# Attention scores with 128 query tokens per matmul where 64 stood, and a logits fold that takes 128 tokens at once

## The chip, the cores and the metric

The kernel runs on one core of a Trainium2 chip. The metric is device time in microseconds (us) of one launch, a median over runs. Every time below is a time of this one core. TensorE (PE) multiplies matrices, VectorE (DVE) and ScalarE (ACT) work on rows, GpSimd (POOL) does what is given to it beside them, SyncE (SP) issues the transfers. TensorE runs at one of two clock levels, 1.2 or 2.4 GHz; the profile gives the granted clock as a share of the higher one.

## The reference

Three layers, one after another, all in float32. The change lies in the first (the scores) and in how the logits of the second are made out of it.

```
# q, k, v: 8 batches, 8 heads, 576 tokens, 64 wide; pool = 8, so 72 keys
k_p = k.reshape(B, H, 72, 8, 64).mean(axis=3);  v_p likewise
scores = matmul(q, k_p.T) / 8;  attn = softmax(scores)
x = matmul(attn, v_p), heads side by side: 4608 tokens x 512
logits = x @ phi                       # 512 x 32 slots
d = softmax(logits, over tokens);  slot_input = d.T @ x
slot_out[e] = relu(slot_input[e] @ w1[e]) @ w2[e]      # 8 experts, 4 slots each
y = softmax(logits, over slots) @ slot_out
h = y @ w_in;  out = (s * relu(h)**2 + b) @ w_out      # 512 -> 2048 -> 512
```

## The kernel before

The attention part works on 36 units. A unit is 128 queries (partitions) times 8 columns of 72 keys. Batches go in pairs of nine units: the first four and the last four are plain units, which hold four heads of two sets of 128 tokens of one batch; the fifth is "mixed" (`is_mixed(U)`), holds 64 tokens of each of the two batches and all 8 heads. So 32 units are plain and 4 are mixed.

A hand-written schedule has STEPS steps. In step n TensorE does, in this order of the program: the fold of the logits of unit n-5 (`fold_logits`, if that unit closes a pair, `closes_logits`), the scores of unit n-1 (L1706 to L1727), the transposes of the queries of unit n (L1751), the logits of unit n-4 (`logits_of`, L1631 or L1626), the transposes of the normalised weights of unit n-3 (L1772), and then pieces of other work: transposes of pooled keys and values (L1543), value times phi (L1566), sums over tokens (L1663, L1668), their turning (L1682) and weighted values (L1691, L1696). Each engine has its own instruction stream; they meet only at semaphores.

What surrounds the scores: ScalarE copies the transposed queries out of PSUM to `qT` (L877), and `qT_kept` lets the scores begin. TensorE needs `sx_ready` of the unit before, since both use the same two PSUM banks `S_B`. When the scores are there (`s_ready`) VectorE takes the maximum (L1191) and subtracts it (L1237), ScalarE takes the exponential (L948), VectorE the sums (L1230) and reciprocals (L1241), GpSimd multiplies (L823), and TensorE transposes (L1772) two steps later.

The score of one head has a contraction of 64 (the head's width), so two heads lie in the upper and lower 64 rows of the array. Before the change each product also takes only 64 of the unit's 128 tokens: `parts()` gives the two halves, `toks` is `0:64` or `64:128`, the result lies in the upper or lower half of a PSUM bank. A plain unit has 4 x 2 x 2 = 16 products, each with 64 rows by 64 columns of stationary data (queries) and 72 moving columns (keys). In the trace every float32 product is two matmul records and two weight-load records, so a unit shows x32. The profile writes such a tile as `64*64`; `128*128` is the full array.

The fold: the logits of unit pairs come out of `logits_of` as four partial sums on four groups of 32 partitions (`l4`, 128 x 256, or 128 x 128 for a mixed unit). `fold` is an identity repeated four times; `l4.T @ fold` adds the four. Before the change it is done for 64 tokens at a time (`128*64`, 32 moving columns): 4 products for a pair, 2 for a mixed unit. VectorE copies the result (L1182).

After the attention (from 193 us of the span) come the experts (L1840, L1864), the hidden layer and its products (L1898 on, the long loop of L1999, L2000, L2010); this part is not touched.

Of the kernel before, what the change touches and what calls it, by code (L numbers as in the profile page):

```python
# [13 lines left out]
P = 128  # L14
# [4 lines left out]
def pooled_attention_soft_moe_squared_relu_kernel(  # L19
# [23 lines left out]
    B, H, S, HD = q.shape  # L43
    D, SLOTS = phi.shape
    EXPERTS, _, F1 = w1.shape
# [3 lines left out]
    KEYS = S // POOL  # L49
    ROW = POOL * HD  # L50
    PER = SLOTS // EXPERTS
    HALF = P // 2
# [18 lines left out]
    HB = H // 2  # L71
# [42 lines left out]
    with ctx:  # L114
        def sb(name, shape, dt=F32, where=ctx):
            return where.enter_context(nc.sbuf_tensor(name, shape, dt))
# [6 lines left out]
        fold = sb("fold", [P, QUADS, SLOTS])  # L123
# [18 lines left out]
        k_sb = {n: sb(f"k_sb{n}", [P, PH, KEYS], where=att)}  # L142
# [6 lines left out]
        qT = sb("qT", [P, HP, P], where=att)  # L149
# [12 lines left out]
        l4 = sb("l4", [P, L4 + P], where=att)  # L162
# [41 lines left out]
        rows = logits[:, :, :].rearrange("p t s -> p (t s)")  # L204
# [30 lines left out]
        Q_B, S_B, A_B, L_B, B_B, MISC = 0, (1, 2), (3, 4), 5, 6, 7  # L235
        bank = []
# [146 lines left out]
        def is_mixed(U):  # L383
            return U % TPP == MIXED

        def unit_half(U):
            u = U % TPP
            return u % 2 if u < MIXED else (u - MIXED - 1) % 2
# [10 lines left out]
        def l4_cols(U):  # L399
            return slice(L4, L4 + P) if is_mixed(U) else slice(0, L4)  # L400

        def logits_closed(U):

            return sum(closes_logits(o) for o in range(U))
# [144 lines left out]
        def parts():  # L549

            return [(bb, slice(HALF * bb, HALF * (bb + 1))) for bb in range(2)]
# [975 lines left out]
        def _(pe):  # L1527
# [71 lines left out]
            def fold_logits(U):  # L1599

                e = logits_closed(U)
                pe.wait_ge(fold_ready, 2)
                pe.wait_ge(l4_kept, e + 1)
                misc_free("logits", e + 1)
                for j in range(1 if is_mixed(U) else 2):
                    for half, toks in parts():
                        first = P * j + HALF * half
                        last = pe.matmul(bank[MISC][toks, SLOTS * j:SLOTS * (j + 1)], l4[:, l4_cols(U)][:, first:first + HALF],
                                         fold[:, 0, :], start=True, stop=True)
                last.then_inc(lg_ready, 1)  # L1610

            def logits_of(U):
# [87 lines left out]
            for n in range(LAST_LOGITS):  # L1700
                U = n - 5
                if 0 <= U < UNITS and closes_logits(U):
                    keep_warm(n, 1)
                    fold_logits(U)

                U = n - 1  # L1706
                if 0 <= U < UNITS:
                    i, bb = U // TPP, unit_batch(U) % 2
                    pe.wait_ge(qT_kept, U + 1)
                    if U % TPP == 0:  # L1710
                        pe.wait_ge(kT_kept, PIECES * (i + 1))
                    if U:
                        pe.wait_ge(sx_ready, U)
                    if is_mixed(U):
                        for h in range(H):
                            rows = slice(HD * (h % 2), HD * (h % 2 + 1))
                            for bb, toks in parts():
                                last = pe.matmul(bank[S_B[h % 2]][toks, KEYS * (h // 2):KEYS * (h // 2 + 1)], qT[rows, h // 2, toks],
                                                 k_sb[i % 2][rows, H * bb + h, :], start=True, stop=True)
                    else:  # L1720
                        for a in range(HB):
                            for j in range(2):
                                rows = slice(HD * j, HD * (j + 1))
                                for _, toks in parts():
                                    last = pe.matmul(bank[S_B[j]][toks, KEYS * a:KEYS * (a + 1)], qT[rows, a, toks],  # L1725
                                                     k_sb[i % 2][rows, H * bb + HB * unit_half(U) + a, :], start=True, stop=True)
                    last.then_inc(s_ready, 1)  # L1727

                for g in groups_at(n, TOP_AT):
                    keep_warm(n, 2)  # L1730
                    turn_tops(g)
                for g in groups_at(n, ROW_AT):
                    keep_warm(n, 1)
                    spread_tops(g)

                U = n
                if U < UNITS:

                    i, w, j = U // TPP, unit_queries(U), unit_tile(U) % TPP
                    if U % TPP in (0, MIXED, MIXED + 1):  # L1740
                        pe.wait_ge(q_in[w], (16, 16, 32)[w] * (i + 1))
                    if n:
                        pe.wait_ge(qT_kept, n)
                        query_bank_free(n - 1)
                    for a in range(HP):
                        if is_mixed(U):
                            src = qbuf[w][:, 2 * a:2 * a + 2, 0, :].rearrange("p h d -> p (h d)")
                        else:
                            j0 = j % (MIXED + 1)
                            src = qbuf[w][:, HB * unit_half(U) + a, j0:j0 + 2, :].rearrange("p j d -> p (j d)")  # L1750
                        last = pe.transpose(bank[Q_B][:, P * a:P * (a + 1)], src, ident[:, :])  # L1751
                    last.then_inc(qT_ready, 1)
                if n == 0:
                    turn_keys(0, 1, 0)
                    turn_keys(0, 2, 0)

                if n == weights_step(0):
                    values_phi(0, n)
                U = n - 4
                if 0 <= U < UNITS:  # L1760
                    keep_warm(n, 1)
                    logits_of(U)

                U = n - 3
                if 0 <= U < UNITS:
                    keep_warm(n, 2)
                    pe.wait_ge(a_ready, U + 1)
                    for g in range(2):
                        if U:
                            pe.wait_ge(aT_kept, 2 * (U - 1) + g + 1)  # L1770
                        for a in range(HB):
                            last = pe.transpose(bank[A_B[g]][0:KEYS, P * a:P * (a + 1)], ex[:, ex_slot(U), HB * g + a, 0:KEYS], ident[:, :])  # L1772
                        last.then_inc(aT_ready, 1)


                if n:
                    for i, u in pieces_with(key_step, n):
                        turn_keys(i, u, n)
                for i, u in pieces_with(value_step, n):
                    turn_values(i, u, n)  # L1780
                for i in range(PAIRS):
                    if i and n == weights_step(i):
                        values_phi(i, n)
                    for half in range(2):
                        if n == natural_step(i, half):
                            values_natural(i, half, n)
                for g, half in b_halves(n):
                    keep_warm(n, half == 0)
                    token_weights(g, half)
                for g in groups_with(bT_step, n):  # L1790
                    keep_warm(n, 1)
                    turn_weights(g)
                for g in groups_with(sums_step, n):
                    keep_warm(n, 1)
                    weighted_values(g)
# [37 lines left out]
            for e in range(EXPERTS):  # L1833
# [4 lines left out]
                for half in range(2):  # L1838
                    for c in range(DC):
                        last = pe.matmul(bank[2 + half][QUAD * c:QUAD * (c + 1), :], sT[:, c, e, :],  # L1840
                                         wv[:, c, BANK * half:BANK * (half + 1)], start=(e == 0), stop=(e == EXPERTS - 1),
                                         skip_group_check=True)
                last.then_inc(matrix_used, 1)
            turn_c(TURN_AT_H)
            for c in range(F1C):
                if c % (F1C // 2) == 0:
                    pe.wait_ge(h_kept, c // (F1C // 2) + 1)
                    pe.wait_ge(h_kept_dve, c // (F1C // 2) + 1)
                last = pe.matmul(bank[6][:, SLOTS * c:SLOTS * (c + 1)], h_sb[:, P * c:P * (c + 1)], fold[:, 0, :],
                                 start=(c == 0), stop=True, skip_group_check=True)  # L1850
            last.then_inc(hT_psum, 1)

            for e in range(EXPERTS):
# [8 lines left out]
                for c in range(F1C):  # L1862
                    quad = c % QUADS
                    last = pe.matmul(bank[4][QUAD * quad:QUAD * (quad + 1), :], hT[:, c, e, :], wv[:, c, :],  # L1864
                                     start=(e == 0 and c < QUADS), stop=(e == EXPERTS - 1 and c >= F1C - QUADS),
                                     skip_group_check=True)
                last.then_inc(matrix_used, 1)
            turn_c(LAST_TURN)
            for c in range(DC):
                if c % (DC // 2) == 0:  # L1870
                    pe.wait_ge(so_kept, c // (DC // 2) + 1)
                last = pe.matmul(bank[5][:, SLOTS * c:SLOTS * (c + 1)], so_sb[:, P * c:P * (c + 1)], fold[:, 0, :],
                                 start=(c == 0), stop=True, skip_group_check=True)
# [190 lines left out]
```

## Time and profile before

| | |
|---|---|
| time, median of 3 runs | 648.23 us (647.69 to 648.74) |
| the profiled execution | 652.14 us, its span 650.3 us |
| mean granted clock | 0.986 |
| PE busy | 629.7 us (97% of the span) |
| DVE, ACT, POOL busy | 481.5, 448.9, 124.2 us |
| scores of plain units (L1725), busy PE | 25.2 us, x1024 |
| folds (L1608), busy PE | 8.0 us, x144 |

The profile counts an engine as busy while at least one of its instructions is in flight. Matmuls of different array tiles run side by side, and the ends of matmuls are modelled, so a sum of durations says little about TensorE; what counts is how far apart the starts lie. The record of a group in a timeline gives the start of its first instruction, the time to the end of its last, and how many records it has. The last 1.8 us of the profiled time lie outside the span.

### The profile page before, as it was taken

The page shows a single profiled execution, that of the slowest core. Times are in us where ns is not written, and L with a number is a line of the kernel's source. Part 1 is how long each engine was busy: PE and PEld are TensorE (multiplying, and loading weights), DVE is VectorE, ACT ScalarE, POOL GpSimd, SP SyncE. Part 2 cuts the span into 40 slices and gives each one's busy share as a digit, 9 for nine tenths or more (in the row PEclk, how much of TensorE's full clock was granted, in tenths as well). Part 3 has the DMA queues.
Part 4 walks back from the last instruction along what each step waited for, and adds up shares of the span by engine and source line. Part 5 has one row for each costly group of instructions (what it writes and reads, how often), then busy time and mean ns, then how long its engine had stood idle before and what let it go on. Part 6 is the DMA issues. An engine that isn't in the chain of part 4 may idle for free.

```text
span 650.3 us, 16686 instructions
## 1 busy us (share of the span) xinstructions
PE 629.7 (97%) x6462; PEld 547.8 (84%) x6462; DVE 481.5 (74%) x796; ACT 448.9 (69%) x754; POOL 124.2 (19%) x126
## 2 busy tenths in 40 slices
PE   7799999999999999999999999999999999999996
PEld 7676776776763347889999999999999999999996
DVE  4888665665535739886888878888888887888876
ACT  1588766676522169996777777777777777777772
POOL 3787887542210010004000000000000000000001
PEclk9699989999999999999999999999999999999999
DMA  9968879386459980001000000000000000000001
GB/s 330 321 196 328 331 236 404 77 329 250 158 206 411 414 366 1 1 1 42 26 34 18 34 16 32 16 32 16 32 16 30 18 32 16 16 32 16 33 18 66
DMA packets 26005, 80.50 MB, mean 124 GB/s; under 512 B 6496, under 2 KB 14688, under 8 KB 23392
## 3 DMA queue, kind: packets, MB, share of 16 engines
q1 hardware_dynamic: 25952, 79.76, 32.9%
q8 instruction: 37, 0.61, 0.4%
q14 instruction: 16, 0.13, 0.1%
HBM read 70.32 MB, written 9.44 MB: 123 GB/s over the span
## 4 chain that ended last, share of the span: by engine, by line
PE 89%; DVE 3%; DMA 2%; POOL 2%; issue 2%; ACT 1%; DVEq 0%; ACTq 0%; POOLq 0%
PE bank L1999 16%; PE bank L2010 16%; PE bank L2000 16%; PE bank L1904 5%; PE bank L1772 5%; PE bank L1725 2%; PE bank L1751 2%; PE bank L1927 2%; PE bank L1631 2%; PE bank L1934 2%; PE bank L1930 2%; PE bank L1864 2%; PE bank L1840 2%; PE bank L1663 2%; DMA kvbuf<-in_v_dram 2%
## 5 line engine op out<-in xcount | busy, mean ns | idle before, releaser
L1388 DVE TENSOR_TENSOR lo_sb<-a_sb,hi_sb 128x896 fp32r<-128x896 f32 x128 | 140.1, 1094 | 57.2 <-PE bank L2010 55.5
L1053 ACT ACTIVATE hi_sb<-a_sb 128x896 fp32r<-128x896 f32 x128 | 122.2, 955 | 77.1 <-PE bank L2000 74.8
L1999 PE MATMUL bank<-w_hi,hi_sb 128*128 128x256 f32 x381 | 96.9, 283 | 0.0
L2000 PE MATMUL bank<-w_lo,hi_sb 128*128 128x256 f32 x381 | 96.9, 283 | 0.0
L1038 ACT ACTIVATE a_sb<-r_sb 128x512 f32<-128x512 f32 x144 | 91.1, 632 | 6.4
L2010 PE MATMUL bank<-w_hi,lo_sb 128*128 128x256 f32 x381 | 87.1, 283 | 0.0
L1031 ACT ACTIVATE r_sb<-bank 128x512 f32<-128x512 f32 x144 | 83.6, 580 | 0.1
L1999 PEld LDWEIGHTS bank<-w_hi,hi_sb 128*128 128x128 f32 x381 | 73.2, 192 | 0.0
L2000 PEld LDWEIGHTS bank<-w_lo,hi_sb 128*128 128x128 f32 x381 | 73.2, 192 | 0.0
L864 POOL TENSOR_TENSOR pu_sb<-pu_sb,logits 128x256 f32<-128x256 f32 x1 | 0.7, 740 | 334.5 <-DVE x_sb L1446 334.5
L1999 PE MATMUL bank<-t_early,hi_sb 128*128 128x256 f32 x256 | 64.3, 283 | 0.0
L2000 PE MATMUL bank<-t_early,hi_sb 128*128 128x256 f32 x256 | 64.2, 283 | 0.0
L2010 PEld LDWEIGHTS bank<-w_hi,lo_sb 128*128 128x128 f32 x381 | 64.0, 192 | 0.0
L1999 PE MATMUL bank<-t_late,hi_sb 128*128 128x256 f32 x252 | 63.2, 283 | 0.0
L2000 PE MATMUL bank<-t_late,hi_sb 128*128 128x256 f32 x252 | 63.2, 283 | 0.0
L972 ACT ACTIVATE aT<-bank 72x512 f32<-72x512 f32 x72 | 38.9, 588 | 20.1 <-PE bank L1772 20.1
L1191 DVE TENSOR_REDUCE mx<-bank 128x8 f32<-128x576 f32 x36 | 27.2, 756 | 34.1 <-PE bank L1725 26.6
L823 POOL TENSOR_TENSOR ex<-ex,den 128x576 f32<-128x576 f32 x36 | 41.4, 1149 | 55.9 <-DVE den L1241 55.9
L1904 PE MATMUL bank<-cT,g_st 128*128 (+1 forms) x256 | 51.5, 283 | 0.0
L1999 PEld LDWEIGHTS bank<-t_early,hi_sb 128*128 128x128 f32 x256 | 49.1, 192 | 0.2
L2000 PEld LDWEIGHTS bank<-t_early,hi_sb 128*128 128x128 f32 x256 | 49.1, 192 | 0.0
L1999 PEld LDWEIGHTS bank<-t_late,hi_sb 128*128 128x128 f32 x252 | 48.4, 192 | 0.0
(213 smaller groups left out, 1333.0 us busy)
## 6 DMA issues: line engine op xcount, KB each, us to landing
early_third<-in_moe_w_dram SPq DMA_DIRECT2D x5, 2048.0 KB, 11.5
kvbuf<-in_k_dram SPq DMA_DIRECT2D x12, 768.0 KB, 5.6
kvbuf<-in_v_dram SPq DMA_DIRECT2D x12, 768.0 KB, 6.1
out_dram<-o_sb SPq DMA_DIRECT2D x36, 256.0 KB, 2.3
qbuf<-in_q_dram SPq DMA_DIRECT2D x8, 1024.0 KB, 7.9
early<-in_moe_w_dram SPq DMA_DIRECT2D x4, 2048.0 KB, 9.9
late<-in_moe_w_dram SPq DMA_DIRECT2D x3, 2048.0 KB, 14.3
after_last<-in_moe_w_dram SPq DMA_DIRECT2D x2, 2048.0 KB, 8.2
```

The lines of the kernel that those rows point to most:

```text
L823: pool.tensor_tensor(e, e, r, ALU.mult).then_inc(a_ready, 1)
L972: act.activation(aT[:, HB * g:HB * (g + 1), :], bank[A_B[g]][0:KEYS, :].rearrange("p (a g) -> p a g", a=HB), ACT.Copy).then_inc(aT_kept, 1)
L1031: act.activation(r_sb[:, n % 2, :], h_bank[:, :], ACT.Relu).then_inc(r_ready, 1)
L1038: act.activation(a_sb[:, n % ARING, 0:CH], r_sb[:, n % 2, :], ACT.Square).then_inc(g_ready, 1)
L1053: act.activation(hi_sb[:, n % 2, :], a_sb[:, n % ARING, P:2 * CH], ACT.Copy).then_inc(hi_ready, 1)
L1191: dve.reduce_max(m, scores, AX.X).then_inc(mx_ready, 1)
L1388: dve.tensor_tensor(lo_sb[:, n % 2, :], a_sb[:, n % ARING, P:2 * CH], hi_sb[:, n % 2, :].bitcast(F32), ALU.subtract).then_inc(lo_ready, 1)
L1772: last = pe.transpose(bank[A_B[g]][0:KEYS, P * a:P * (a + 1)], ex[:, ex_slot(U), HB * g + a, 0:KEYS], ident[:, :])
L1904: last = pe.matmul(bank[7][:, PAIR * i:PAIR * (i + 1)], g_st[:, P * f:P * (f + 1)], cT[:, bass.ds(c * PAIR + CH, PAIR)], start=True, stop= ...
L1999: pe.matmul(acc, hi, rhs_hi, start=(k == 0 and (at == AT1 or at % 2 == 1)), stop=False, skip_group_check=True)
L2000: last = pe.matmul(acc, hi, rhs_lo, start=False, stop=False, skip_group_check=True)
L2010: last = pe.matmul(half_bank(odd, at), lo_sb[:, n % 2, P * lhs:P * (lhs + 1)], rhs_hi, start=False, stop=(k == KP - 1), skip_group_check=True)
```

## The change

The loops over `parts()` go away at two places. In the scores of plain units the stationary operand is all 128 tokens (`qT[rows, a, :]`), the result fills all partitions of the bank: 8 products of 64 rows by 128 columns in place of 16 of 64 by 64, with the same 72 moving columns. In the fold it is `P * j:P * (j + 1)`: 2 products (1 for a mixed unit) of 128 by 128 with 32 moving columns in place of 4 (2) of 128 by 64. The scores of mixed units (L1718) keep their 16 products of 64 by 64, since their two halves need different keys.

```diff
@@ fold_logits
                 for j in range(1 if is_mixed(U) else 2):
-                    for half, toks in parts():
-                        first = P * j + HALF * half
-                        last = pe.matmul(bank[MISC][toks, SLOTS * j:SLOTS * (j + 1)], l4[:, l4_cols(U)][:, first:first + HALF],
-                                         fold[:, 0, :], start=True, stop=True)
+                    last = pe.matmul(bank[MISC][:, SLOTS * j:SLOTS * (j + 1)], l4[:, l4_cols(U)][:, P * j:P * (j + 1)],
+                                     fold[:, 0, :], start=True, stop=True)
@@ scores of plain units
                             for j in range(2):
                                 rows = slice(HD * j, HD * (j + 1))
-                                for _, toks in parts():
-                                    last = pe.matmul(bank[S_B[j]][toks, KEYS * a:KEYS * (a + 1)], qT[rows, a, toks],
-                                                     k_sb[i % 2][rows, H * bb + HB * unit_half(U) + a, :], start=True, stop=True)
+                                last = pe.matmul(bank[S_B[j]][:, KEYS * a:KEYS * (a + 1)], qT[rows, a, :],
+                                                 k_sb[i % 2][rows, H * bb + HB * unit_half(U) + a, :], start=True, stop=True)
```

TensorE's stream of instructions in the steps of units 5 and 6, before (a size is stationary columns by moving columns; `x16` counts products, each of which is two records in the trace):

```order
 L1543 MATMUL bank<-ident,kp 128x128 x3
-L1608 MATMUL bank<-fold,l 64x32 x4
-L1725 MATMUL bank_2<-k_sb,qT 64x72 x16
-L1751 MATMUL bank<-ident,qbuf 128x128 x4
-L1631 MATMUL bank<-aT,vphi 32x256 x4
-L1772 MATMUL bank<-ident,ex 72x128 x8
+L1606 MATMUL bank<-fold,l 128x32 x2
+L1722 MATMUL bank_2<-k_sb,qT 128x72 x8
+L1748 MATMUL bank<-ident,qbuf 128x128 x4
+L1629 MATMUL bank<-aT,vphi 32x256 x4
+L1769 MATMUL bank<-ident,ex 72x128 x8
```

Nothing has changed its place; line numbers have moved by two and three. The fold has half the products at twice the stationary columns, and so have the scores. The other engines' streams are the same as before.

## Rows read from the trace of the kernel before

**Rows 1.** Windows: busy us (and records) per engine, then clock, DMA share, GB/s

```profile
core 0: us, PE busy (x) PEld busy (x) DVE busy (x) ACT busy (x) POOL busy (x), PEclk, DMA share, GB/s
28.10:50.80 22.70, 20.42 (x386) 15.61 (x385) 18.47 (x33) 17.63 (x36) 19.48 (x20) 1.00 0.67 213
50.80:89.50 38.70, 36.88 (x674) 27.20 (x674) 26.66 (x57) 29.08 (x61) 30.85 (x31) 1.00 0.86 304
89.50:93.00 3.50, 3.50 (x26) 3.26 (x22) 2.79 (x6) 1.98 (x5) 3.50 (x4) 0.51 0.44 90
93.00:171.50 78.50, 75.10 (x1393) 55.74 (x1393) 47.17 (x105) 55.68 (x117) 37.40 (x37) 1.00 0.66 245
193.00:241.00 48.00, 47.30 (x369) 17.77 (x369) 29.04 (x53) 14.98 (x30) 1.95 (x2) 1.00 1.01 415
```

**Rows 2.** Waits of PE, 50.8 to 171.5 us: total, times, longest

```profile
PE bank L1608 <- issue: 1.3, 1, 1.3
PE bank L1646 <- issue: 0.9, 1, 0.9
PE bank L1725 <- issue: 0.9, 1, 0.9
PE bank L1718 <- issue: 0.8, 1, 0.8
PE bank L1751 <- ACT k_sb L884: 0.4, 2, 0.2
...
PE bank L1751 <- ACT vT L893: 0.2, 1, 0.2
```

**Rows 3.** Groups by line and shape, PE, 50.8 to 171.5 us

```profile
L1725 PE MATMUL bank<-k_sb,qT 64*64 64x72 f32 x768 | 17.9, 229 | 0.9 <-issue 0.9
```

**Rows 4.** Timeline of PE, 106.2 to 110 us: start, us to the last end

```profile
107.18 0.43 PE L1608 MATMUL bank<-fold,l 128*64 128x32 f32 x8
107.54 0.73 PE L1725 MATMUL bank<-k_sb,qT 64*64 64x72 f32 x32
108.20 0.66 PE L1751 MATMUL bank<-ident,qbuf 128*128 128x128 f32 x4
```

**Rows 5.** Instructions of single lines: duration ns min/median/max, first and last start

```profile
L1725 PEld LDWEIGHTS bank<-k_sb,qT x1024: 129/133/228, 14.8 to 169.6; 64*64 64x64 f32 x171
L1751 PEld LDWEIGHTS bank<-ident,qbuf x144: 137/141/229, 12.7 to 166.1; 128*128 128x128 f32 x144
L1591 PEld LDWEIGHTS bank<-ident x46: 186/192/247, 172.3 to 192.6; 128*128 128x128 f32 x46
L1591 PE MATMUL bank<-ident x46: 275/275/377, 172.3 to 192.7; 128*128 128x128 f32 x46
```

**Rows 6.** Timeline of PE, 208.9 to 232 us, matmuls with `fold` as moving operand

```profile
209.77 1.94 PE L1849 MATMUL bank<-fold,scratch 128*128 128x32 f32 x16 [0.30 <-DVE scratch L1323]
...
230.75 1.08 PE L1872 MATMUL bank<-fold,scratch 128*128 128x32 f32 x8
```

**Rows 7.** Timeline of PE, 14 to 60 us

```profile
19.71 1.24 PE L1725 MATMUL bank<-k_sb,qT 64*64 64x72 f32 x32
...
36.56 0.49 PE L1543 MATMUL bank<-ident,kp 128*128 128x128 f32 x3
36.99 0.42 PE L1608 MATMUL bank<-fold,l 128*64 128x32 f32 x8
...
48.04 0.31 PE L1608 MATMUL bank<-fold,l 128*64 128x32 f32 x4
```

**Rows 8.** Windows between three stops of PE named issue; columns as rows 1

```profile
103.25:111.78 8.53, 8.17 (x122) 5.32 (x123) 5.20 (x11) 5.68 (x11) 5.21 (x6) 1.00 1.02 403
111.78:119.15 7.37, 6.44 (x124) 4.93 (x123) 3.45 (x8) 4.37 (x9) 5.06 (x6) 1.00 0.86 253
```

**Rows 9.** Chain that ended last, 14 to 50.8 us: start, length

```profile
41.42 1.15 POOL ex L823
42.57 1.78 POOL kvbuf L803
...
47.84 1.77 POOL kvbuf L803
```

## The prediction

> **What bounds the kernel now.** I read the windows first. From 50.8 to 171.5 us TensorE is busy for 36.88 of 38.70, then 3.50 of 3.50, then 75.10 of 78.50 us, while VectorE, ScalarE and GpSimd have a fifth or more of the time free in most of it [rows 1]. Next the waits of TensorE in that stretch: the four longest are "issue" (3.9 us together), stops in which no semaphore holds it; for ScalarE's key and value copies it waits 0.6 us [rows 2]. So from 50.8 us on, the time of the attention part is the sum of what TensorE puts through, and a tenth of a microsecond more in a step is a tenth more at the end. Before 50.8 us that isn't so: GpSimd is busy for 19.48 of 22.70 us [rows 1] and the chain runs through its pooling and normalising [rows 9]. After 193 us the experts and the hidden layer follow on TensorE (47.30 of 48.00 us busy) [rows 1]; they begin when the attention ends and take over its delay whole. Their loads wait for TensorE's progress and are delayed with it, so they aren't late for the first time.
>
> **Scores, the main term.** What a matmul costs here is the distance from its start to the next, and two things can set it: the moving columns streamed, and the load of the stationary columns for the next one, which runs beside the matmul in flight. Now: 32 records take 0.73 us [rows 4]. They go in 8 rounds of four array tiles (two halves of rows, two of columns). The last record lasts 0.22, the first load shows as 0.05, four tiles are staggered by 0.02 in all: 0.44 us for 7 distances, 0.063 us a round.
>
> After: 16 records in 8 rounds of two tiles, each 64 rows by 128 columns. The moving columns stay at 72 and would still allow 0.063. The load doesn't: 64 columns take 133 ns, 128 plain columns 192 ns [rows 5]. What distance such a load permits is shown by matmuls with 128 stationary and only 32 moving columns: 16 in 1.94 us, the last one 0.28 long, so 1.66 / 15 = 0.111 us; and between 8 records in 1.08 and 16 in 1.94 it is 0.86 / 8 = 0.108 [rows 6]. There the load is the bound, and I take 0.111. The first round waits about 0.10 for its load in place of 0.05: a keep-warm matmul that finds nothing loaded shows 377 against 275 ns [rows 5].
>
> A unit then takes 0.10 + 7 x 0.111 + 0.01 + 0.22 = 1.11 us in place of 0.73: plus 0.38. The stretch from 50.8 us has 768 of these records, 24 units [rows 3]: 24 x 0.38 = **9.1 us**. No trace row has a 64-by-128 tile. From below, if loads as short as those of the transposes applied (141 ns for 128 columns [rows 5]), the round could stay at 0.063 and the term is 0. From above, if the loads of the two row halves took turns, it is 15 x 0.111 in place of 7, 0.89 more a unit, 30 us in all. The nearest row decides: the four loads of a round now run side by side (0.063 a round, though each takes 133 ns), and a plain load's length follows its columns.
>
> The Trainium skill (TensorEngine Tiling (Array Packing), Theoretical Speedup) gives up to twice the speed for each dimension at or below 64 that is tiled. By that rule giving up the column tiling costs a factor of two in the score matmuls, rounds of 0.126: 24 x (0.05 + 7 x 0.063) = 11.8 us for this term. The rows say a factor of 1.76, as the load and not the lost tile is what binds, and I keep 9.1; with 11.8 the whole would be 661.4, still inside the forecast's own range.
>
> **Folds.** A pair's fold is now 8 records in 0.43 us; a mixed one 4 in 0.31 [rows 4, 7], so 0.06 a round of two. After, 4 records: 0.10 + 3 x 0.111 + 0.22 = 0.66; mixed, 2 records: 0.43. Where a narrow tile precedes (L1668, L1696: 8 pair folds and 3 mixed ones in the stretch) that is 8 x 0.23 + 3 x 0.12 = 2.2 us. Where a full-width stage precedes (6 more), the array now has to run empty first: the last of three transposes starts near 36.78, the fold at 36.99, 0.20 later [rows 7]. The new fold is full-width too and follows at 0.11, its load hidden: 0.09 and 0.10 saved of 0.23, about 0.05 each, 0.3 us. Sum **2.5 us**; bounds 1 and 3.5.
>
> **Units before 50.8 us.** Eight plain units. At the lower clock level a unit takes 1.24 us [rows 7]; with everything twice as slow its cost is about 0.7. Two such units lie on the chain, and one warm one at most; the rest hides behind GpSimd [rows 9], whose cover of 3 us in 22.7 is thin. I take **1.7 us**, bounds 0.5 and 4.2 (nothing hidden).
>
> **What is given back.** The 0.6 us in which transposes of queries wait for ScalarE's copies [rows 2], and some 0.2 us of the same before 50.8, are covered by longer scores: **-0.8 us** (bounds 0 and -1.2). And the stops named issue: three of them are 245 and 247 records apart [rows 8], with nothing else in common, one even amid a group of the same line. I read them as TensorE's own instructions arriving late by the block. The change removes 32 of a unit's 64 score records, 0.8 thousand of some 4.2 thousand in the stretch, so there are fewer blocks, and the bursts of 64 records within 0.7 us that empty the queue become 32 in 1.1. Of 3.9 us I take half as gone, **-2.0 us**; bounds 0 and -3.9. I can't say where the new blocks end.
>
> **Sum.** 9.1 + 2.5 + 1.7 - 0.8 - 2.0 = 10.5 us. On the profiled execution, 652.1, it gives 662.6; that one is 3.9 above the median of the runs, to which the sum is added as well: 648.2 + 10.5 = **658.7 us**. Two of three terms rest on one number, the 0.111 of a 128-column load.
>
> VectorE gets each unit's scores 0.38 later in the step. It needs them for the maximum and the subtraction, and the next unit's scores wait for the latter; they start some 4 us after the scores before, and the two take 1.5 us, so this doesn't bind. Behind VectorE's longer wait stand only the sums of the unit before and GpSimd's multiply, whose result is used a step later.
>
> **Rivals.**
> - Wide loads cost nothing in 64-row tiles (the other side). Place: the rounds of the scores. For it: the transposes load 128 columns in 141 ns. Against: every plain load of 128 columns takes 192, at f32 as here. Scores and folds then cost nothing and only the fewer instructions count, 2 to 4 us: 645 us. It decides the sign if a round stays under about 0.075 us (8 x 24 x 0.012 = 2.3 us, what is given back). 6%. The Trainium skill (TensorE: Matmul & The Clock Gate, Weight-path perf modes) has a fast load for 128 stationary columns but not for float32, so by that rule it doesn't help here; the row of 192 ns agrees.
> - Mostly absorbed: all stops of issue vanish (-3.9), and the slow-clock stretch at 89.5 us, 3.5 us at 0.51 [rows 1], goes too, as it follows right on the longest stop (-1.7); of the early units only 0.5 counts. 9.1 + 2.5 + 0.5 - 0.8 - 3.9 - 1.7 = 5.7: 654 us. For it: one idle cause lies behind both. Against: it needs every block to end well. 15%.
> - More time at the lower clock: fewer matmul records in flight, and three stretches more as that of rows 1, 1.7 us each, on top: 664 us. For it: such a stretch is there after one stop of 1.3 us. Against: stops of 0.9 in busy surroundings had none, and TensorE is not more idle after the change. 6%.
> - The two row halves load by turns: 9.1 becomes 30, 680 us. Against: the four tiles' loads overlap today. 3%.
> - The forecast, 656 to 662: 70%.
>
> **Numbers.** A measurement here tells a change of 0.2%, 1.3 us, from none. Slower by more: the forecast, absorbed, clock and turns, all but a tail of the absorbed case: 0.92. Faster: 0.05. Within: 0.03. The range for 8 in 10 goes from 652.5 (absorbed, with fold and early terms at their lower bounds) to 665.5 (no stop gone, early units in full).
>
> **What would show it.** Scores of a plain unit: x16, about 1.1 us, loads of 190 ns, starts 0.11 apart between rounds; if 0.063, the first rival; if 0.22, the last. Folds: x4 in 0.66 or, after full-width work, near 0.6. The first expert matmul, now at 193.1 us, at about 203.5. Experts and the loop after it unchanged in length. VectorE's wait for scores longer by 0.38 a unit. I am wrong if the stretch from 50.8 us grows by under 5 us, or if time comes after 193 us.

## The result and the profile after

| | before | after |
|---|---|---|
| time, median | 648.49 us (4 runs, 647.69 to 649.03) | 656.58 us (4 runs, 655.89 to 659.72) |
| ratio after / before | | 1.0147, interval 1.0121 to 1.0173 |
| profiled execution, its span | 652.14, 650.3 us | 656.41, 654.5 us |
| PE busy | 629.7 us | 639.7 us |

The change makes the kernel 8.1 us slower. Forecast were 10.5, a time of 658.7 us in a range of 652.5 to 665.5. The profiled executions lie only 4.3 us apart (652.14 and 656.41), since that of the kernel before was one of its slower ones. The windows of the changed kernel (busy us and records of each engine, clock, DMA share, GB/s), to be read beside [rows 1]:

```profile
52.36:89.50 37.14, 37.14 (x494) 29.12 (x490) 25.45 (x55) 27.08 (x57) 27.02 (x28) 1.00 0.84 298
89.50:93.00 3.50, 3.50 (x50) 2.38 (x43) 2.05 (x5) 2.29 (x6) 3.42 (x3) 1.00 0.52 193
93.00:175.40 82.40, 82.40 (x1114) 64.23 (x1112) 49.12 (x110) 56.98 (x121) 41.34 (x41) 1.00 0.64 237
197.50:245.50 48.00, 47.39 (x368) 17.86 (x369) 29.02 (x52) 15.08 (x30) 1.95 (x2) 1.00 1.01 416
```

TensorE has no idle time at all from 52.4 to 175.4 us: 82.40 busy of 82.40. The waits and stops of [rows 2] have gone, and so has the stretch at half clock at 89.5 us. The part after 197.5 us is as before, only later: the first expert matmul starts at 197.5 us in place of 193.1. A timeline of TensorE, the place that answers to [rows 4] (start, length to the last end):

```profile
108.66 0.63 PE L1606 MATMUL bank<-fold,l 128*128 128x32 f32 x4
109.22 1.11 PE L1722 MATMUL bank<-k_sb,qT 64*128 64x72 f32 x16
110.27 0.66 PE L1748 MATMUL bank<-ident,qbuf 128*128 128x128 f32 x4
```

Sixteen score records take 1.11 us where thirty-two took 0.73, and the fold 0.63 where it took 0.43. The single instructions (duration ns min/median/max) show why; compare the 133 ns in [rows 5]:

```profile
L1722 PEld LDWEIGHTS bank<-k_sb,qT x512: 182/188/334, 14.9 to 173.8; 64*128 64x128 f32 x171
L1722 PE MATMUL bank<-k_sb,qT x512: 272/272/486, 14.9 to 173.9; 64*128 64x72 f32 x171
```

And the early part, beside [rows 7]:

```profile
19.76 1.99 PE L1722 MATMUL bank<-k_sb,qT 64*128 64x72 f32 x16
...
37.69 0.49 PE L1543 MATMUL bank<-ident,kp 128*128 128x128 f32 x3
38.02 0.53 PE L1606 MATMUL bank<-fold,l 128*128 128x32 f32 x4
```

At half clock a unit takes 1.99 against 1.24 us. After a full-width stage the fold starts 0.33 after it (38.02 - 37.69) where it was 0.43 (36.99 - 36.56). That fits the prediction's reading that the array no longer has to run empty in between.

### The profile page after: what moved, and what is told of

The parts are those of the page before. It is cut to its first block, busy times and chain, and to the rows that moved or that the text cites. A ratio compares the mean times of both kernels' runs of the same rounds, so it can differ in the third digit from the quotient of the medians.

```text
span 654.5 us, 15518 instructions
## 1 busy us (share of the span) xinstructions
PE 639.7 (98%) x5878; PEld 560.8 (86%) x5878; DVE 481.4 (74%) x796; ACT 448.7 (69%) x754; POOL 124.3 (19%) x126
## 4 chain that ended last, share of the span: by engine, by line
PE 93%; DVE 3%; DMA 2%; POOL 1%; issue 1%; ACT 0%; DVEq 0%; ACTq 0%
PE bank L1996 16%; PE bank L2007 16%; PE bank L1997 16%; PE bank L1722 5%; PE bank L1769 5%; PE bank L1901 5%; PE bank L1748 3%; PE bank L1629 3%; PE bank L1924 2%; PE bank L1931 2%; PE bank L1927 2%; PE bank L1861 2%; PE bank L1837 2%; DMA kvbuf<-in_v_dram 2%; PE bank L1661 2%; PE bank L1606 1%
```

## The experiments

The kernels were timed in three sessions (four rows of the table each), each session beside the kernel before on the same chip. The kernel before had there 647.37 us (23 runs, 644.76 to 650.35), 647.57 (645.41 to 652.39) and 647.56 us (645.39 to 651.87).

| kernel | median us (least to most, runs) | ratio to before, interval | profiled execution |
|---|---|---|---|
| before_again | 647.83 (644.39 to 650.70, 12) | 1.0012, 0.9989 to 1.0034 | 647.40 |
| scores_only | 654.40 (654.18 to 654.90, 6) | 1.0103, 1.0080 to 1.0127 | 654.21 |
| fold_only | 649.84 (647.68 to 651.15, 12) | 1.0037, 1.0019 to 1.0055 | 647.68 |
| after_again | 656.92 (656.04 to 657.87, 6) | 1.0139, 1.0115 to 1.0164 | 656.87 |
| before_warm | 651.02 (649.47 to 653.83, 12) | 1.0048, 1.0023 to 1.0073 | 650.71 |
| after_warm | 653.31 (653.19 to 655.51, 6) | 1.0086, 1.0052 to 1.0120 | 653.34 |
| before_wide | 650.66 (649.58 to 656.60, 13) | 1.0045, 1.0025 to 1.0066 | 656.60 |
| after_wide | 655.49 (654.11 to 656.64, 6) | 1.0114, 1.0080 to 1.0149 | 654.37 |
| before_shift64 | 654.23 (650.11 to 657.12, 6) | 1.0096, 1.0065 to 1.0128 | 650.11 |
| before_shift128 | 653.54 (648.86 to 656.91, 12) | 1.0078, 1.0053 to 1.0104 | 650.21 |
| after_shift64 | 656.48 (655.80 to 657.58, 6) | 1.0123, 1.0096 to 1.0149 | 657.58 |
| before_warm256 | 647.54 (645.64 to 651.55, 12) | 0.9995, 0.9972 to 1.0017 | 648.06 |

**The two halves of the change.** Neither kernel needs a diff of its own: scores_only takes the second hunk of the change, fold_only the first, before_again and after_again are the two kernels unchanged.

> The kernel before, unchanged, profiled once more. Theory A (the profiled execution of before, 652.1 us, lost some 4 us to stops named issue and to a 3.4 us stretch at the lower clock which the timed executions, 648.2, lost only in part): this profile shows a span near 646 to 648, at most three stops of 0.5 us or more between 51 and 172 us, and no stretch at 0.5 of the clock there. Theory B (stops and slow stretch belong to every execution of this kernel, and the profile is longer for another reason): five stops again at the same places, span 650.

> Only the scores take 128 tokens per product; the fold stays at 64. Theory A (a round of two 64x128 tiles is bound by the load of 128 stationary columns, 0.105 us against 0.063; 24 units in the full stretch and part of 8 before it): 32 records of 0.73 us become 16 of 1.11, and the time is 5 to 8 us above before. Rival (the longer time is mainly the fold's): under 3 us above before.

> Only the fold takes 128 tokens at once; the scores stay at 64. Theory A (three loads of 128 columns on the path, 0.2 us a pair fold after a narrow stage, nearly nothing after a full-width one): 1.5 to 2.5 us above before. Rival (it is hidden, or its fewer instructions pay for it): within 0.5 us of before. If the two edits add up, this and scores_only together make the 8.1 us of the whole change.

> The changed kernel once more, beside the two halves of the change on one chip: 656 to 657 us, 7.5 to 8.5 us above before. Theory A on the stops: again none of 0.5 us or more between 52 and 179 us, so that it is a property of the kernel and not of one execution; the rival (stops fall by chance) expects two or three of them here.

Measured beside 647.4 us of before: 7.0, 2.5 and 9.6 us (differences of medians). The halves add up, 9.5 against 9.6. The scores are the larger part, as theory A had it. The 9.6 is more than the 7.5 to 8.5 expected; beside 647.4 to 648.5 us of before, the change cost 8.1, 9.6 and 8.9 us in three sets of runs (the last with after_shift64, below). The fit of the halves is in part luck: fold_only also takes records out of TensorE's stream, and its profile has stops of 0.9 us in all where before_again's has 2.2, and the same span within 0.1 us (645.7 and 645.6). Before's second profile has three stops named issue where the first had five; waits of PE between 51.3 and 164.7 us (total, times, longest):

```profile
PE bank L1725 <- issue: 0.9, 1, 0.9
PE bank L1718 <- issue: 0.8, 1, 0.8
PE bank L1608 <- issue: 0.5, 1, 0.5
```

Its span is 645.6 us and nothing there is at half clock. The first profiled execution, 652.1 us, was a dear one, as theory A said. It matters for the reading of any pair: the two first profiles lie 4.2 us apart, and the medians 8.1. after_again and scores_only have no stop in this stretch; their six executions each also spread less, 1.8 and 0.7 us against 5.6 of the 23 of before in that session (the first four of the changed kernel spread by 3.8). All six profiles with wide scores are free of such stops, and all eight with narrow ones have two or more: the stops are a matter of the kernel.

**What binds a round of tiles.** Three of the four heads' products get 120 moving columns in place of 72; the surplus lies where the next head's product then writes. `keys` holds the unit's four heads side by side; after_wide has the same edit with all 128 tokens.

```diff
-                                    last = pe.matmul(bank[S_B[j]][toks, KEYS * a:KEYS * (a + 1)], qT[rows, a, toks],
-                                                     k_sb[i % 2][rows, H * bb + HB * unit_half(U) + a, :], start=True, stop=True)
+                                    base = H * bb + HB * unit_half(U)
+                                    keys = k_sb[i % 2][rows, base:base + HB, :].rearrange("d a k -> d (a k)")
+                                    wide = KEYS * a + (120 if a < HB - 1 else KEYS)
+                                    last = pe.matmul(bank[S_B[j]][toks, KEYS * a:wide], qT[rows, a, toks],
+                                                     keys[:, KEYS * a:wide], start=True, stop=True)
```

> The kernel before, but the score products of the first three of a unit's four heads have 120 moving columns in place of 72 (the surplus is overwritten by the next head's product, results unchanged). Theory A (rounds of 64x64 tiles are bound by the moving columns): transposes with 128 moving columns start 0.109 apart and these scores with 72 at 0.063, so 120 give 0.102; 6 of 8 rounds grow by 0.04, 0.24 us a unit, 5 to 8 us on the whole. Rival (bound by issue or by loads): within 1 us of before.

> The changed kernel with the same 120 moving columns. Theory A (a round of 64x128 tiles is bound by the load of 128 stationary columns, 0.105 to 0.111 us, in which 120 moving columns at 0.102 fit): within 1 us of the changed kernel's 656.9, units stay at 1.11 to 1.15 us. Rival (moving and loading add up in the wide tiles): 0.24 us a unit more, 662 us or above.

Timeline of TensorE in before_wide, and then in after_wide:

```profile
107.08 0.97 PE L1728 MATMUL bank<-k_sb,qT 64*64 64x120 f32 x32
```

```profile
107.20 1.11 PE L1725 MATMUL bank<-k_sb,qT 64*128 64x120 f32 x16
```

With the narrow tiles the unit grows from 0.73 to 0.97 us, the 0.24 that moving columns as the bound give: its rounds start 0.103 us apart, and 0.063 with 72 columns. With the wide tiles it stays at 1.11, with rounds 0.112 apart in both: two thirds more moving columns cost no time. The moving columns don't bind the wide tiles, then. The pace is that of the fold's full-width products, 0.112 apart with only 32 moving columns, and what these have in common with the wide scores is the plain load of 128 columns. This settles what the prediction took from a distant row. The whole times are a poorer measure. before_wide is 3.1 us above before, less than the 5 to 8 expected, and after_wide 1.4 below the changed kernel, where 1 was expected. The profiled execution of after_wide has only 3.4 us of half clock in the early part where the changed kernel has 13.7; more array work before and in that part would explain it, which wasn't tried apart. The executions of after_wide agree with that: the three at a mean granted clock of 0.996 take 654.1 to 654.6 us, the three at 0.989 to 0.992 take 656.4 to 656.6, as the changed kernel does. For before_wide the median granted clock is 0.994 against 0.990 of before. By my estimate that is 5 us less at half clock, worth some 2.6 us (of a stretch at half clock half is lost), and would put it near the 5 to 8; no run tested this. Its profiled execution is its slowest (656.6), with one stop of 3.05 us:

```profile
91.33 0.43 PE L1608 MATMUL bank<-fold,l 128*64 128x32 f32 x4 [3.05 <-issue]
91.69 1.72 PE L1728 MATMUL bank<-k_sb,qT 64*64 64x120 f32 x32
```

The scores right after the stop take 1.72 in place of 0.97 us: half clock from 90.1 us on, for 6.8 us. Such a stop is paid for twice, but not every long stop is: half clock came with the stops of 1.31 us (before), 1.46 (before_warm, below) and 3.05, and not with those of 1.54 (before_warm256), 1.82 (before_shift64) and 2.38 us (before_shift128).

**The half clock in the early part.** Products of the identity fill TensorE's idle time between 11 and 22 us. `FILL` gives their number by step, behind the transposes of the queries (`...` stands for lines left out):

```diff
-    START_WARM = 7
+    START_WARM = 14
+    FILL = {0: 4, 1: 10, 2: 3}
...
+                for _ in range(FILL.get(n, 0)):
+                    pe.matmul(bank[A_B[0]][:, 0:P], ident[:, :], ident[:, :], start=True, stop=True)
```

> The kernel before, with matmuls of the identity (7 + 4 + 10 + 3 products, result unused) in the places where TensorE stands idle between 11 and 22 us of the span. Theory A (before's executions differ, 644 to 651 us, since TensorE is at half clock for 6.8 or for 13.7 us from about 15 us on, and this follows on its idle time there): no stretch at half clock before 100 us, unit 9 starts its scores at 50.5 us or earlier (52.1 and 51.3 in the two profiles of before), the time is 644 to 647 us and spreads less. Rival (the early part is bound by GpSimd and transfers alone, the clock costs nothing): unit 9 at 51.3 us as before, 647 us and more, the same spread.

> The changed kernel with the same added matmuls. Theory A: no early stretch at half clock, three units cost 1.11 in place of 1.99 us, so 2 to 3.5 us less than the changed kernel's 656.9: 653.5 to 655. The distance to before_warm is then the pure cost of the change without the clock, 7.5 to 9.5 us. Rival: 656 to 657, early part hidden.

after_warm is as theory A had it, 653.3 us, 3.6 less than the changed kernel; window of after_warm, clock in the third column from the right:

```profile
14.40:28.50 14.10, 12.96 (x140) 11.43 (x138) 10.94 (x15) 7.41 (x16) 11.20 (x11) 1.00 1.06 372
```

and of the changed kernel, with the early stretch at half clock:

```profile
14.80:28.50 13.70, 11.82 (x73) 9.79 (x74) 8.82 (x12) 4.66 (x10) 9.03 (x9) 0.50 1.01 346
```

Unit 9 starts its scores at 50.7 us there, at 53.7 in the changed kernel. before_warm falls against both theories: it is slower than before, 651.0 us, and its unit 9 starts at 53.6 us (of the rival only "647 us and more" holds). So the distance of the two warm kernels is 2.3 us and not the 7.5 to 9.5 expected of it. Its early stretch is at full clock too, and its unit 5 starts at 34.7 us (37.3 in the first profile of before). But then TensorE stops for 1.46 us at 41.1 us, half clock follows for 6.8 us, and more stops come (timeline of TensorE in before_warm):

```profile
41.11 1.11 PE L1752 MATMUL bank<-ident,qbuf 128*128 128x128 f32 x4 [1.46 <-issue]
...
80.63 0.72 PE L1726 MATMUL bank<-k_sb,qT 64*64 64x72 f32 x28 [0.84 <-issue]
```

Its 24 products are 96 records, so they also move all that follows in TensorE's stream. This asked for the third set. I counted all instructions of TensorE's stream in order of time (loads, matmuls, and its semaphore and register instructions) and took the number of the load behind each stop. In before, before_again, fold_only, before_warm and before_wide all stops named issue after 30 us lie at numbers that leave 193 when divided by 256 (2497, 3009, 3265, 3521 and 4801 in the first profile), whatever the work there was.

The transfers say the same. The profile of before has a DMA queue named instruction (packets, MB, share):

```profile
q8 instruction: 37, 0.61, 0.4%
```

That is 16 KB a packet, and in this stretch there is one for each 256 records. In the first profile the packets before the five stops begin at 85.03, 100.76, 109.33, 116.33 and 151.35 us, and TensorE goes on at 87.45, 103.30, 111.80, 119.18 and 153.61, each time 2.3 to 2.8 us later. At the places of 256 records without a stop the packet began 2.8 to 7.0 us ahead. In the two profiles of the changed kernel between 54 and 166 us it is 3.5 to 9.0 us ahead each time. So a stop is a transfer of instructions that began too late. What makes it begin late isn't shown.

**The place of the blocks.** Tiny products in an idle time near 11 us move all that follows in the stream, and no work in time: unit 0 starts its scores at 14.85 and 14.63 us, where before has 14.86.

```diff
+            for x in range(16):
+                at = QUAD * (x % QUADS)
+                pe.matmul(bank[A_B[0]][at:at + QUAD, 0:1], ident[:, 0:QUAD], ident[:, 0:1], start=True, stop=True)
```

before_shift128 has `range(32)`. before_warm256 has the fill of before_warm, but as 7 full and 57 quarter-width products (`FILL = {0: 16, 1: 40, 2: 1}`), 256 records in all.

> The kernel before with 16 tiny products (32 stationary, 1 moving column; 64 records) in TensorE's idle time near 11 us, so that every later instruction stands 64 records further on in the stream. Theory A (TensorE's instructions come in blocks of 256 records, and stops fall where a block is late: in all profiles so far the stops named issue lie at record numbers that leave 193 when divided by 256): the stops are again at such numbers, so at other places of the work, and their sum and the time may differ from before by up to 3 us either way. Rival (stops belong to the work or to the transfers beside it): they stay at the same work, now at numbers that leave 1, and the time stays.

> The same with 32 tiny products, 128 records. Theory A: stops at numbers that leave 193, yet another set of places; with the kernel before and the shift by 64 it gives the spread that a placement of blocks is worth, 1 to 4 us between best and worst. Rival: all three the same within 0.5 us.

> The changed kernel with the 16 tiny products. Theory A (half the records in a score burst, so the next block is there in time wherever it begins): no stop over 0.5 us between 52 and 179 us, time within 1 us of the changed kernel, 656 to 657.5. Rival (the changed kernel is free of stops by a lucky placement): stops appear, 658 to 660.

> The kernel before with matmuls of the identity in TensorE's idle time from 11 to 22 us, 64 products, 256 records in all, so that the blocks of the later instructions stay where they are in the kernel before. Theory A: no early stretch at half clock (or a shorter one), the stops of before at its own places, 1 to 3 us less than before, 644.5 to 646.5: better than both kernels. Rival (added matmuls delay the early part, as before_warm with 651.0 may suggest): 648 us or more.

Stops in before_shift64, timeline of TensorE:

```profile
78.81 0.47 PE L1728 MATMUL bank<-k_sb,qT 64*64 64x72 f32 x12 [0.85 <-issue]
86.65 0.30 PE L1629 MATMUL bank<-aT,vphi 72*32 72x64 f32 x3 [1.82 <-issue]
142.19 0.47 PE L1728 MATMUL bank<-k_sb,qT 64*64 64x72 f32 x14 [1.16 <-issue]
```

and in before_shift128:

```profile
70.17 0.46 PE L1721 MATMUL bank<-k_sb,qT 64*64 64x72 f32 x11 [0.77 <-issue]
...
119.19 0.47 PE L1728 MATMUL bank<-k_sb,qT 64*64 64x72 f32 x13 [0.84 <-issue]
141.44 1.06 PE L1566 MATMUL bank<-phi_bd,vT 128*72 128x64 f32 x14 [2.38 <-issue]
```

All six leave 193 again (2241, 2497, 4545; 1985, 3777, 4545), and so do the other stops of these profiles and of before_warm256 (30 stops in the eight profiles, without an exception). They fall at other work than in before: theory A. The stream comes in blocks of 256 and TensorE stops where one is late. The Trainium skill (Runtime: NRT & Kernel Launch, Instruction fetch mechanics) says that instructions are fetched in blocks of 256 and that crossing into the next is "mostly hidden"; the block agrees with the spacing here, the hiding holds in the profiles with wide scores and not in those with narrow ones, where one crossing cost up to 3.05 us.

The size surprised: 16 products of no use cost the kernel before 6.7 us (654.2 against 647.6), twice what I had allowed, and 32 of them 6.0. The changed kernel isn't moved by them: 656.5, no stop, though at one place (72.8 us) the packet began only 2.4 us ahead. So the kernel before sits at a favourable place of its blocks, and against before_shift64 the change costs 2.3 us, not 8 or 9. before_warm, moved by 96 records, fits in between with 651.0. The profiled executions of the shifted kernels are near their fastest (650.1 and 650.2), and where the further 3 to 4 us of the others go is known in part. The median granted clock of all their executions is 0.986 against 0.990 of before, and their profiled ones had 0.988 and 0.990. By my estimate the 0.986 means 5 to 6 us more at half clock than before has, worth some 3 of the 6.7 and 6.0 us. before_warm256 is where before is, 647.5, between the two theories: its median clock is 0.9965, and it gains nothing by it. In its profile GpSimd binds at 25.5 us, 3.4 us of half clock follow, and unit 9 starts at 52.06 us, as in the first profile of before (52.10). One of its two stops after 50 us lies at the work of one of before's, the other doesn't. Against it after_warm, both filled, is 5.8 us slower. No kernel tried beats the one before.

## Why the prediction was right

The cleanest pair are the profiles of before_again and of the changed kernel, 8.85 us apart in span (645.61, 654.46), near the distance of the medians. Starts of the same groups on TensorE, paired one by one, give each term (a stop counts here with all that the next group starts later by):

| step | predicted | measured in this pair |
|---|---|---|
| scores, 24 units | +9.1 | +9.2 (0.38 each) |
| folds in the stretch and the tail | +2.5 | +2.3 (0.21 each; 0.09 net after full-width stages) |
| before unit 9 | +1.7 | +2.3 |
| waits for copies, covered | -0.8 | -1.3 |
| stops named issue (measured: with a wait of 0.35 for GpSimd) | -2.0 | -3.7 |
| sum | +10.5 | +8.8 |

**Scores.** Right to the hundredth: 1.11 us a unit, loads of 188 ns, rounds 0.112 apart (0.111 was taken from the full-width rows). Two small parts of that sum were off and cancelled: the last record lasts 0.27 us and not 0.22, and the first round costs 0.055 us more than a later one, as in the narrow tiles, and not 0.10. before_wide and after_wide show that the bound has changed sides, from moving columns to the load. The factor of two that I weighed beside it would be 0.126 a round.

**Folds.** 0.63 us against 0.66; the sum holds. fold_only is 2.5 us slower than before, which agrees, but its blocks lie elsewhere too.

**Early units.** The mechanism held. The +2.3 of this pair has a longer stretch at half clock in it: that lasted 13.7 us in both profiles of the changed kernel and in that of scores_only, 13.7 and 6.8 in those of before. Where both had 13.7, in the two first profiles, unit 9 starts at 52.10 and 53.68 us, +1.6 beside the forecast 1.7. TensorE was busy for 1.59 of 4.90 us before the shorter one began (windows of before_again):

```profile
14.40:19.30 4.90, 1.59 (x38) 1.30 (x39) 3.46 (x3) 1.07 (x3) 3.94 (x4) 1.00 1.08 327
19.30:26.10 6.80, 6.02 (x81) 4.44 (x80) 4.66 (x9) 3.67 (x8) 5.05 (x5) 0.52 1.09 368
```

Whether wide scores cause the longer stretch or it fell so, these profiles don't decide; over all executions the mean granted clock is hardly lower, median 0.989 (16 of the changed kernel) against 0.990 (69 of before). after_warm prices it for the changed kernel: 3.6 us.

**Given back.** This is the term that was mis-sized. I took half of 3.9 us of stops as gone; all went. In before_again the stops show as 2.2 us of idle time, but by the starts they and two delays with hardly any idle time cost some 3.4. That fewer blocks and slower bursts would leave fewer stops was right, and the six profiles with wide scores, that of after_shift64 among them, show that it isn't luck. (The 245 and 247 records of [rows 8] are blocks of 256: the rest are semaphore and register instructions.) What I missed is that the kernel before, as timed, was itself lucky: its stops depend on where in the work its blocks begin. Against the two shifted placements the change costs 2.3 and 2.9 us, and there my rival "mostly absorbed" (5.7) would have been nearest. For the second of these I assume that a shift by 128 leaves the changed kernel where it is; only 64 was tried.

**Where luck came in.** Measured from the profiled execution of before on which the terms were read, the forecast is missed: 662.6 us was the sum, 656.4 came. Between these two profiles the stretch from unit 9 to the experts grows by 2.8 us, under the 5 that I had named as a sign of being wrong, and the first expert matmul starts at 197.5 and not at 203.5. Scores and folds are as forecast there too, but all stops go (some 6 us by the starts) and with them the half clock at 89.5 us (1.7): the terms of "mostly absorbed". The medians came out at 8.1 because the executions of before, as timed, mostly lose less to stops and clock than that one did; with before_again the same stretch grows by 6.6.

## What to carry to other kernels

Count for a matmul both its moving columns and the stationary columns of the next load; tiles of 64 columns were close to balance here (0.063 us a round with 72 moving columns in the scores, 0.059 with 32 in the fold), and doubling the stationary side of a two-row tile put the load on the path at once. Halving the number of instructions is worth something by itself where a dense stretch has none to spare, but in this kernel its worth depended on where the blocks of 256 began: before believing a difference of 1%, move the stream by a few dozen useless instructions and time again. A profile is one execution; take a second one of the same kernel before subtracting.

## What the runs showed of the hardware, not expected

- Sixteen products without use, in idle time, made this kernel 6.7 us slower (before_shift64, 1.0096, interval 1.0065 to 1.0128), though none of its work is later at the start.
- 64-by-128 tiles, with 72 or 120 moving columns: two loads of 128 columns at different rows run side by side; a round takes 0.112 us, as one full-width load does.
- Stops without a semaphore lie only at places 256 records apart and end 2.3 to 3.0 us after a transfer of 16 KB in the queue named instruction began: 30 of 30 in eight profiles.
- Half clock came during or within 2.1 us after stops of 1.31, 1.46 and 3.05 us, and not with stops of 1.54, 1.82 and 2.38 us.
